# The first batch's down projection of a finished tile, issued two attention units later on TensorE

## The chip, the core and the metric

The kernel runs on one core of a Trainium2 chip. The time is the device time of one execution in microseconds; lower is better. One execution of the kernel before was also recorded by the hardware profiler, and all rows below come from that one.

## The reference

Sliding-window attention with four sink keys, over 2 batches, 8 heads, 768 positions and head size 64, is followed by two token-and-channel mixers. All data is fp32.

```python
keep = is_sink | in_window                       # 4 sinks, window of 128
scores = where(keep, q @ k.T / sqrt(D), -1e9)
a = exp(scores - max); a = a / (sum(a) + 1e-09)
x = a @ v                                        # -> (B, 768, 512)
# first mixer
h = x.T @ U @ V                                  # U: 768 x 32, V: 32 x 768
u = x + h.T
x = u + relu(u @ w_ch1) @ w_ch2
# second mixer
h = relu(x.T @ w_tok1) @ w_tok2
u = x + h.T
out = u + relu(u @ w_ch1) @ w_ch2
```

The "down projection" of this change is the first product of the first mixer, `x.T @ U`, summed over the positions.

## The kernel before

**Tiles and units.** The positions are cut into tiles of 128 rows: six tiles (T = 0 to 5) for the first batch and six for the second. One attention unit is one head of one tile, numbered u = 8 T + h. For the first batch the function `attention(0)` writes, unit by unit, what is issued. In unit u TensorE computes the scores of head u (three products, line 1185), the product of probabilities and values "pv" of head u - 4 (line 1212, four matmul instructions), and the transposes of the probabilities "probsT" of head u - 2 (line 1193). So three heads are in flight. In a unit with h = 0 the queries of the next tile are transposed first, in one with h = 2 its keys (line 1170).

**The other engines in a unit.** VectorE adds the mask and takes the maximum (line 951). ScalarE takes the exponential (line 800). GpSimd copies the sink columns (line 718). The transposed probabilities are copied from PSUM to SBUF, into `probs_T`, by VectorE for even heads (line 962) and by ScalarE for odd ones (line 808). pv of a head waits for that copy.

**The end of a tile.** The last pv of tile T - 1 is issued in unit h = 3 of tile T, and the sink product that completes its output (line 1221) in unit h = 4. VectorE then adds a small number to the eight row sums (line 973), takes reciprocals (line 975) and multiplies the output by them into `x_nat` (line 978). In the same unit VectorE has, ahead of this, the rounding of the next tile's keys (line 935, not in T = 5, where it comes later) and the mask of head 4, and behind it the copy of the transposed probabilities of head 2. At tile T = 3 two more steps on `V_sb` (lines 984 and 987) stand between line 978 and that copy. GpSimd computes the low part of the keys, `k_lo` (line 501), at about the same time.

**The down projection.** In unit h = 5 of tile T, behind everything else of the unit, TensorE multiplies the finished tile T - 1 by U (line 1230, one f32 product that the hardware runs as two weight loads and two matmuls). It waits for `x_nat` of that tile (line 1229). The six products of the first batch add up in one PSUM bank; only the last is followed by anything on another engine (lines 762 and 899). That last one, for tile 5, comes after all attention units of the batch.

**Order of the work.** The list `plan` holds one order for all engines; each engine walks it and issues its own part of each step. The step `("down", 1, 0, t)` with t below 5 makes TensorE issue its product and makes no other engine, and no DMA queue, do anything. PSUM banks, semaphore values and DMA issues are derived from the same list.

**After the attention.** From about 81 us of the span to its end TensorE does the channel products of the mixers, with the second batch's attention put between them.

Of the kernel before, what the change touches and what calls it, by code (L numbers as in the profile page):

```python
# [5 lines left out]
def attention_then_two_mixers(  # L6
# [57 lines left out]
    def attention(b):  # L64

        lo, hi = b * NQ * H, (b + 1) * NQ * H
        units, late = [], []
        LAG_T, LAG_V = LAGS[b]
        for u in range(lo, hi + LAG_V):
            T, h = divmod(u, H)  # L70
            now, scores, probsT, pv = [], [], [], []
            if u == 0:
                now += [("qT", T), ("kT", T), ("qsplit", T), ("ksplit", T)]
            if lo <= u - LAG_V < hi and (u - LAG_V) % H == H - 1:
                now.append(("sinksT", (u - LAG_V) // H))
            if u == hi and T < NTILES:
                now.append(("ksplit", T))
            if u == hi + 1 and T < NTILES:
                now.append(("ksplit_odd", T))
            if u < hi and T + 1 < NTILES:  # L80
                if h == 0:
                    now.append(("qT", T + 1))
                if h == (2, 1)[b]:
                    now += [("kT", T + 1), ("qsplit", T + 1)]
                if h == 4 and T + 1 < hi // H:
                    now.append(("ksplit", T + 1))
                if h == 6 and T + 1 < hi // H:
                    now.append(("ksplit_odd", T + 1))
            if u < hi:
                scores.append(("scores", u))  # L90
            if lo <= u - LAG_T < hi:
                probsT.append(("probsT", u - LAG_T))
            if lo <= u - LAG_V:
                pv.append(("pv", u - LAG_V))
            sinkpv = [("sinkpv", (u - LAG_V) // H)] if lo <= u - LAG_V and (u - LAG_V) % H == H - 1 else []
            if b == 0 and u < hi + LAG_V - 1:
                pv, late = late + pv, sinkpv
            elif b == 0:
                pv = pv + late + sinkpv
            now += scores + pv + probsT  # L100
            if b == 0 and h == 5 and T > 0:
                now.append(("down", 1, b, T - 1))
            units.append(now)
            if b and sinkpv:
                units.append(sinkpv)
        return units
# [73 lines left out]


    plan = [s for unit in attention(0) for s in unit] + [("down", 1, 0, NQ - 1)]
    waiting = attention(1) + preparation(1, 1)
    for n, s in ((24, ("wload", 0)), (23, ("wload", 1)), (19, ("wsum", 0)), (16, ("wsplit", 0)), (11, ("wsum", 1)),
                 (11, ("wload", 2))):
# [1200 lines left out]
```

How the kernel before makes its waits and increments, by code:

```python
        def wait_drained(eng, s):  # L520
            kind, at = s
            if kind == "qT":
                eng.wait_ge(q_copied, at + 1)
            elif kind == "kT":
                eng.wait_ge(k_copied, at + 1)
            elif kind == "sinksT":
                eng.wait_ge(psinkT_ready, at + 1)
            elif by_act(at):
                eng.wait_ge(probsT_by_act, (at + 1) // 2)
            else:
                eng.wait_ge(probsT_by_dve, at + 1 - (at + 1) // 2)
# [1 line left out]
        def wait_used(eng, c):  # L534
            s = chunks[c][0]
            if s[0] == "mm1":
                eng.wait_ge(m_ready, m_at[s, 0] + 1)
            elif s[0] == "up":
                eng.wait_ge(m_ready, m_at[s[:4], KD - 1] + 1)
            elif s[0] == "down" and s[3] == NQ // 2 - 1:
                eng.wait_ge(m_ready, m_at[s[:3], KG - 1] + 1)
            elif s[0] == "mm2" and ends(s):
                eng.wait_ge(m_ready, m_at[s[:4], TPH - 1] + 1)
            else:
                eng.wait_ge(chunk_done, chunk_count[c])
# [33 lines left out]
            def load_qk(T):  # L580
                if T >= 2:
                    sp.wait_ge(tp_ready, tp_at["kT", T - 2] + 1)
                sp.dma_start(q_nat[:, T % 2, :].rearrange("p (h d) -> p h d", h=H), heads(q, T)) \
                  .then_inc(q_loaded[T % 2], 16)
                sp.dma_start(k_nat[:, T % 2, :].rearrange("p (h d) -> p h d", h=H), heads(k, T)) \
                  .then_inc(k_loaded[T % 2], 16)
```

## Time and profile before

| what | value |
|---|---|
| median of 3 runs | 655.9 us (655.68, 655.9, 657.08) |
| the profiled execution, its own time | 657.41 us |
| its span, first to last instruction | 655.6 us |
| TensorE busy with matmuls | 631.2 us, 96% of the span |
| mean granted TensorE clock | 0.997 |
| first batch's attention, up to its last down projection | about 81 us |

The profiled execution is 1.81 us longer than its span; that is what lies around the first and last instruction. It is 1.5 us longer than the median of the three runs. The span shows which engine waited for which, in rows that give a start, a length and, in brackets, the idle time of the engine just ahead of the instruction with what ended it. The granted clock is a share of 2.4 GHz.

### The profile page before, as it was taken

To read this page: it belongs to the slowest core of one execution; us is meant where nothing else is said; L and a number is where in the kernel's file an instruction comes from. 1 tells how busy PE (TensorE), PEld (TensorE's weight loads), DVE (VectorE), ACT (ScalarE), POOL (GpSimd) and SP (SyncE) were. 2 spreads that over 40 slices of the span, in tenths; PEclk is the share of its full clock that TensorE was granted. 3 is DMA by queue.
4 is the path that set the end of the run, shared out by engine and by line. 5 is a ranking of instruction groups with operands and counts; after the bars stand their busy time and mean duration, and the time that the engine had idled before them with its cause. 6 is when DMAs were issued, how large, how long until landed. Compare 5 with 4: busy or idle time off the path is not lost.

```text
span 655.6 us, 10345 instructions
## 1 busy us (share of the span) xinstructions
PE 631.2 (96%) x3532; PEld 565.9 (86%) x3532; DVE 336.7 (51%) x733; ACT 316.2 (48%) x707; POOL 367.0 (56%) x373
## 2 busy tenths in 40 slices
PE   6888999999999999999999999999999999999998
PEld 5878888889888987799999988889998888899986
DVE  7776552433333254276757562186758325676411
ACT  4655575455444553464545444364544445554321
POOL 8544366656464656246656745375656543757262
PEclk9998999999999999999999999999999999999999
DMA  8344244433324425223232243233232343431142
GB/s 182 85 93 113 50 129 118 110 102 108 97 67 107 148 65 146 64 67 110 81 106 88 70 135 101 81 112 97 81 108 87 103 136 98 134 94 47 49 130 95
DMA packets 88276, 65.51 MB, mean 100 GB/s; under 512 B 43008, under 2 KB 72192, under 8 KB 88224
## 3 DMA queue, kind: packets, MB, share of 16 engines
q1 hardware_dynamic: 88224, 64.85, 35.0%
q8 instruction: 29, 0.48, 0.3%
q14 instruction: 23, 0.19, 0.1%
HBM read 61.42 MB, written 3.15 MB: 98 GB/s over the span
## 4 chain that ended last, share of the span: by engine, by line
PE 87%; DVE 5%; ACT 3%; POOL 2%; issue 2%; DMA 0%; DVEq 0%; ACTq 0%; POOLq 0%
PE bank L1356 33%; PE bank L1155 21%; PE bank L1322 10%; PE bank L1212 4%; PE bank L1185 4%; PE bank L1193 3%; PE bank L1286 3%; PE bank L1249 2%; PE bank L1230 2%; PE bank L1170 1%; PE bank L1263 1%; POOL w_lo L753 1%; ACT w_hi L774 1%; PE bank L1348 1%; DVE x_nat L978 1%
## 5 line engine op out<-in xcount | busy, mean ns | idle before, releaser
L753 POOL TENSOR_TENSOR w_lo<-w_raw,w_hi 128x512 fp32r<-128x512 f32 (+1 forms) x158 | 205.9, 1309 | 170.5 <-ACT w_hi L774 170.0
L774 ACT ACTIVATE w_hi<-w_raw 128x512 fp32r<-128x512 f32 (+1 forms) x158 | 96.3, 618 | 61.0 <-PE bank L1356 43.0
L1155 PE MATMUL bank<-b_hi,a_hi 128*128 128x384 f32 x280 | 94.8, 338 | 1.0 <-DVE temps L1065 0.6
L1155 PE MATMUL bank<-b_lo,a_hi 128*128 128x384 f32 x280 | 94.8, 339 | 0.0
L1356 PE MATMUL bank<-w_hi,hid_hi 128*128 128x512 f32 x216 | 87.6, 406 | 0.0
L800 ACT ACTIVATE probs<-masked,neg_max 128x264 f32<-128x264 f32 x96 | 49.5, 516 | 74.3 <-DVE neg_max L951 73.8
L1356 PE MATMUL bank<-w_hi,hid_lo 128*128 128x512 f32 x216 | 85.1, 394 | 0.0
L1356 PE MATMUL bank<-w_lo,hid_hi 128*128 128x512 f32 x216 | 84.7, 392 | 0.0
L1356 PE MATMUL bank<-w_hi,y_hid 128*128 128x512 f32 x216 | 71.1, 394 | 0.2
L951 DVE CUSTOM_DVE_ANT_0 masked<-bank,masks 128x264 f32<-128x264 f32 x96 | 41.2, 430 | 39.4 <-PE bank L1185 35.5
L718 POOL COPY p_sink<-probs 128x12 f32<-128x12 f32 x96 | 19.3, 202 | 69.8 <-ACT probs L800 68.2
L896 DVE SCALAR_TENSOR_TENSOR hid_lo<-bank,hid_hi 128x384 fp32r<-128x384 f32 x32 | 17.8, 557 | 76.9 <-ACT hid_hi L762 76.9
L1155 PEld LDWEIGHTS bank<-b_hi,a_hi 128*128 128x128 f32 x280 | 52.6, 188 | 3.4 <-POOL a_lo_odd L743 1.0
L1155 PEld LDWEIGHTS bank<-b_lo,a_hi 128*128 128x128 f32 x280 | 52.7, 188 | 1.6
L1212 PE MATMUL bank<-v_nat,probs_T 128*128 128x64 f32 x352 | 51.1, 264 | 1.2 <-ACT probs_T L808 0.7
L1212 PEld LDWEIGHTS bank<-v_nat,probs_T 128*128 128x128 f32 x352 | 48.8, 193 | 2.9 <-ACT probs_T L808 1.8
L1356 PEld LDWEIGHTS bank<-w_hi,y_hid 128*128 128x128 f32 x216 | 40.5, 188 | 9.5 <-POOL w_lo L753 1.5
L1356 PEld LDWEIGHTS bank<-w_hi,hid_lo 128*128 128x128 f32 x216 | 40.5, 188 | 9.0
L1155 PE MATMUL bank<-b_hi,a_lo_even 128*128 128x384 f32 x140 | 47.3, 338 | 0.0
L1155 PE MATMUL bank<-b_hi,a_lo_odd 128*128 128x384 f32 x140 | 47.1, 336 | 0.0
L1356 PEld LDWEIGHTS bank<-w_lo,hid_hi 128*128 128x128 f32 x216 | 40.7, 188 | 7.2 <-issue 0.5
L1356 PEld LDWEIGHTS bank<-w_hi,hid_hi 128*128 128x128 f32 x216 | 40.7, 188 | 6.8 <-POOL w_lo L753 0.3
(137 smaller groups left out, 1410.0 us busy)
## 6 DMA issues: line engine op xcount, KB each, us to landing
w_raw<-in_moe_w_ch_dram SPq DMA_DIRECT2D x144, 256.0 KB, 2.7
w_raw<-in_moe_w_ch_dram SPq DMA_DIRECT2D x20, 512.0 KB, 3.5
q_nat<-in_q_dram SPq DMA_DIRECT2D x12, 256.0 KB, 3.0
k_nat<-in_k_dram SPq DMA_DIRECT2D x12, 256.0 KB, 3.7
v_nat<-in_v_dram SPq DMA_DIRECT2D x12, 256.0 KB, 3.4
out_dram<-o_stage SPq DMA_DIRECT2D x12, 256.0 KB, 3.6
w_raw<-in_moe_w_tok_dram SPq DMA_DIRECT2D x6, 256.0 KB, 2.7
w_raw<-in_moe_w_tok_dram SPq DMA_DIRECT2D x8, 192.0 KB, 2.3
```

Source lines behind the costliest of these rows:

```text
L718: nc.gpsimd.tensor_copy(p_sink[:, T % 2, :].rearrange("p (c n) -> p c n", c=3)[:, :, N_SINK * h:N_SINK * (h + 1)], probs[:, u % 4, P:BLK]. ...
L753: nc.gpsimd.tensor_tensor(w_lo[:, split % NW, 0:n], w_raw[:, split % NR, 0:n], w_hi[:, split % NW, 0:n].bitcast(f32), ALU.subtract) \
L774: nc.scalar.activation(w_hi[:, split % NW, 0:n], w_raw[:, split % NR, 0:n], ACT.Copy) \
L800: nc.scalar.activation(probs[:, u % 4, :], masked[:, u % 3, :], ACT.Exp, bias=neg_max[:, u % (2 * H):u % (2 * H) + 1], scale=-1.0, accum_o ...
L951: nc.vector.tensor_tensor_reduce(out=masked[:, u % 3, :], in0=s_slots(u)[0][:, 0:NK], in1=masks[:, mask_of(T), :], scale=1.0, scalar=3.0e3 ...
L1155: last = mm(bank[:, 0:HALF], w[at % 2][:, a, k, :], u[:, b_part, k, :], start=(first and n == 0), stop=(n == 5), skip_group_check=True)
L1185: last = mm(bank[:, 0:NK], qs[:, T % 2, h // 2, :], keys(ks, T, h // 2, h % 2), start=(n == 0), stop=(n == 2))
L1193: last = nc.tensor.transpose(tp_banks[tp_bank_of[s]][:, j * P:(j + 1) * P], probs[:, u % 4, col:col + P], ident[:, :])
L1212: last = mm(o_bank(T)[:, h * D:(h + 1) * D], probs_T[:, u % 2, j * P:(j + 1) * P], v_nat[:, tile % 3, h * D:(h + 1) * D], start=(h == 0 an ...
L1286: last = mm(m_tile((s[:4], d))[:, 0:HALF], tok[:, g, rows], w[:, slot, 0:HALF], start=False, stop=(g == KG - 1 and n == 2), skip_group_che ...
L1322: last = mm(m_tile(use)[:, 0:HALF], w[:, slot, rows], u[:, kk, cols], start=(n == 0), stop=(n == 3 * KD - 1))
L1356: last = mm(m_tile(use)[:, :], stationary, w[:, slot, :], start=False, stop=(final and n == 2), skip_group_check=True)
```

## The change

The step `("down", 1, 0, T - 1)` is appended to unit h = 7 of tile T in place of unit h = 5. It concerns the five products for tiles 0 to 4, issued during tiles 1 to 5. The sixth keeps its place. Nothing else is edited.

```diff
             now += scores + pv + probsT
-            if b == 0 and h == 5 and T > 0:
+            if b == 0 and h == 7 and T > 0:
                 now.append(("down", 1, b, T - 1))
             units.append(now)
```

## Rows read from the trace of the kernel before

**Rows 1.** The page: TensorE's busy time; shares of the chain that ended last.

```profile
PE 631.2 (96%) x3532; PEld 565.9 (86%) x3532; DVE 336.7 (51%) x733; ACT 316.2 (48%) x707; POOL 367.0 (56%) x373
...
PE 87%; DVE 5%; ACT 3%; POOL 2%; issue 2%; DMA 0%; DVEq 0%; ACTq 0%; POOLq 0%
```

**Rows 2.** Waits of TensorE, 0 to 185 us: total us, times, longest.

```profile
PE bank L1230 <- DVE x_nat L978: 5.4, 5, 1.4
```

**Rows 3.** Timeline of tile 2, units 5 to 8: start, length, engine, line, operands.

```profile
34.68 1.27 POOL L501 TENSOR_TENSOR k_lo<-uT_full,k_hi 64x512 fp32r<-64x512 f32 x1
...
34.80 1.18 DVE L973 TENSOR_SCALAR sums_eps<-sums 128x8 f32<-128x8 f32 x1
...
35.26 0.39 PE L1193 MATMUL bank<-ident,probs 128*128 128x128 f32 x2
...
36.25 0.69 DVE L978 TENSOR_TENSOR x_nat<-bank,recip 128x512 f32<-128x512 f32 x1
36.86 0.41 DVE L962 COPY probs_T<-bank 128x256 f32<-128x256 f32 x1
...
36.99 1.10 PE L1230 MATMUL bank<-x_nat,U_sb 128*96 128x512 f32 x2 [1.35 <-DVE x_nat L978]
...
38.17 0.36 ACT L808 ACTIVATE probs_T<-bank 128x256 f32<-128x256 f32 x1
...
38.30 0.55 PE L1212 MATMUL bank<-v_nat,probs_T 128*128 128x64 f32 x4
...
38.69 0.39 PE L1193 MATMUL bank<-ident,probs 128*128 128x128 f32 x2
...
39.28 0.55 PE L1212 MATMUL bank<-v_nat,probs_T 128*128 128x64 f32 x4
...
39.67 0.39 PE L1193 MATMUL bank<-ident,probs 128*128 128x128 f32 x2
...
39.90 0.60 PE L1170 MATMUL bank<-ident,q_nat 128*128 128x128 f32 x4
```

**Rows 4.** Timeline of tile 5, from unit 5, and the units behind it.

```profile
72.65 0.39 PE L1193 MATMUL bank<-ident,probs 128*128 128x128 f32 x2
...
74.10 0.55 PE L1212 MATMUL bank<-v_nat,probs_T 128*128 128x64 f32 x4
...
76.69 0.66 PE L1212 MATMUL bank<-v_nat,probs_T 128*128 128x64 f32 x4 [0.21 <-ACT probs_T L808]
...
77.19 0.39 PE L1193 MATMUL bank<-ident,probs 128*128 128x128 f32 x2
...
78.76 0.19 PEld L1221 LDWEIGHTS bank<-v_sink,p_sinkT 96*128 96x128 f32 x1 [0.19 <-DVE p_sinkT L967]
```

**Rows 5.** Timeline of tile 1, units 5 to 8.

```profile
24.37 0.39 PE L1193 MATMUL bank<-ident,probs 128*128 128x128 f32 x2
...
25.10 0.41 DVE L962 COPY probs_T<-bank 128x256 f32<-128x256 f32 x1
...
26.41 0.36 ACT L808 ACTIVATE probs_T<-bank 128x256 f32<-128x256 f32 x1
...
28.20 0.60 PE L1170 MATMUL bank<-ident,q_nat 128*128 128x128 f32 x4
```

**Rows 6.** Timeline of tile 4, unit 5.

```profile
62.68 1.10 PE L1230 MATMUL bank<-x_nat,U_sb 128*96 128x512 f32 x2 [1.35 <-DVE x_nat L978]
```

**Rows 7.** Timeline of tile 3, units 5 and 6.

```profile
48.68 1.10 PE L1230 MATMUL bank<-x_nat,U_sb 128*96 128x512 f32 x2 [1.32 <-DVE x_nat L978]
...
50.10 0.42 DVE L962 COPY probs_T<-bank 128x256 f32<-128x256 f32 x1
...
50.58 1.07 PE L1212 MATMUL bank<-v_nat,probs_T 128*128 128x64 f32 x4 [0.43 <-DVE probs_T L962]
```

**Rows 8.** Stretches with busy us (count) of each engine, granted clock, DMA share, GB/s.

```profile
50.60:50.70 0.10, 0.10 (x1) 0.10 (x1) 0.10 (x1) 0.00 (x0) 0.00 (x0) 0.78 0.00 0
...
54.00:54.10 0.10, 0.10 (x2) 0.10 (x1) 0.00 (x0) 0.10 (x1) 0.10 (x1) 0.66 0.00 0
```

## The prediction

> **What bounds the kernel now.** I read the page first. TensorE is busy for 96% of the span and makes up 87% of the chain that ended last [rows 1], so the time changes only where TensorE gains or loses idle time. The list of TensorE's waits comes next: the down projection of line 1230 waits for VectorE's `x_nat` for 5.4 us in five places, the largest single entry of the attention stage [rows 2]. One of the five is the last product (tile 5's), which does not move. The other four are in tiles 1 to 4. In tile 5 there is no wait. It looks as if moving the product behind two more units frees some 4.5 us. Whether it does is to be read from the timeline around each place: what does TensorE meet next when it no longer stops there?
>
> **One place in full: tile 2 [rows 3].** VectorE works in order. It finishes `x_nat` at 36.94 (36.25 + 0.69), and directly behind it stands the copy of the transposed probabilities of head 2, from 36.86 to 37.27. TensorE has ended unit 5 with the transposes at 35.26 and waits from there for `x_nat`, until 36.99. But the pv of head 2 is in unit 6, and it needs that copy. So with the product gone from unit 5, TensorE issues the three score products of unit 6 and then stops for the copy, which comes 0.33 us after the `x_nat` that it had waited for. The wait changes its name and place, and the product that stood beside VectorE's work no longer does.
>
> Step by step. The distance from one unit's transposes to the next pv is 0.59 us (38.69 to 39.28). From a pv that did not wait to its unit's transposes it is 0.39 (38.30 to 38.69). From a pv that waited it is 0.50 (76.69 to 77.19 [rows 4]). Where the down projection stands between transposes and pv, the distance is 1.45 (72.65 to 74.10 [rows 4]); it costs 1.45 - 0.59 = 0.86 us of TensorE when nothing waits. TensorE resumes 0.05 us after the end of what it waited for (36.94 to 36.99).
>
> - Before: pv of head 2 at 38.30, pv of head 3 at 39.28, transposes at 39.67, next tile's queries at 39.90 [rows 3].
> - After: the natural time for pv of head 2 is 35.26 + 0.59 = 35.85; the copy allows 37.27 + 0.05 = 37.32. Its transposes are at 37.82. The pv of head 3 could start at 38.41, but it needs ScalarE's copy, which ends at 38.53 (38.17 + 0.36). That copy is not earlier than before: it stands behind the exponential of head 5, and this behind the mask that VectorE does after the copy of head 2. So pv of head 3 is at 38.58, its transposes at 39.08, then the down projection, and the queries at 39.08 + 0.23 + 0.86 = 40.17, where 0.23 is the distance 39.67 to 39.90.
>
> That is 0.27 us later than before. The bounds: if resuming costs nothing over the plain 0.39, it is 0.05; if ScalarE's and VectorE's copies each came another 0.2 late, some 0.5.
>
> **The other four places.**
> - Tile 4 has the same wait of 1.35 us and the same pattern [rows 6]: +0.27.
> - Tile 1 [rows 5]: VectorE's copy ends at 25.51, so pv of head 2 at 25.56, transposes 26.06, pv of head 3 naturally at 26.65, by ScalarE's copy (26.41 + 0.36) at 26.82, transposes 27.32, queries at 28.41. Before they were at 28.20: +0.21.
> - Tile 3 [rows 7]: here even the kernel before waits for the copy, 0.43 us behind the down projection and the scores, and starts pv at 50.58. The product is wholly beside VectorE's work. After the change pv still starts at 50.58, and the 0.86 us come on top: +0.86. At half clock it would be up to 1.7, but see below.
> - Tile 5 [rows 4]: no wait for `x_nat`, so nothing is gained or uncovered in unit 5. The product moves into the thin units behind unit 47, which have no scores and some short waits: 0.21 us for ScalarE's copy at 76.69, and 0.19 for the sink product's weights at 78.76. If both are filled the end is 0.4 earlier. But the last heads' copies and the sink chain move with the scores, and I find only the first part usable: -0.1. On the other side all of 0.86 could come on top.
>
> Nothing else moves: no other engine and no DMA queue issues anything for these steps. The load of queries and keys waits for transposes that shift by 0.3 us at most per tile. From 81 us on TensorE is the bound until the end, so what is lost by then stays.
>
> Sum: 0.21 + 0.27 + 0.86 + 0.27 - 0.1 = +1.5 us. Its ends, place by place, are about +0.8 and +2.7. Against the profiled execution's own time: 657.41 + 1.5 = 658.9.
>
> **The clock, and the median.** TensorE's granted clock falls to one half (1.2 GHz) at 50.66 and is back to 2.4 GHz at 54.07 [rows 8]. Ahead of it TensorE was idle for 1.32 us, worked for about 1.5, and was idle for 0.43 [rows 7]. In this stretch of 3.41 us TensorE has work all the time, so the fall costs about half, 1.7 us (1.7 of 655.6 is also all that the mean clock of 0.997 leaves room for, so it is the only fall). The profiled execution lies 1.5 us above the median 655.9, and one of the three runs (657.08) lies 1.2 above it. I read this as runs with the fall and runs without it. After the change TensorE has, from 48.68 - 1.32 = 47.36 on, only the three score products of unit 6 (some 0.4 us) before 50.58: one idle stretch of 2.8 us, where there were two with work between. I expect the fall in most runs, no longer in some. Then the median goes from a run without to a run with it: 655.9 + 1.5 + 1.2 to 1.5 gives 658.6 to 658.9. A fall that begins during the idle time costs less, since a part of it is spent waiting; I take 658.5. If half or more of the runs are spared, the median is 655.9 + 1.5 = 657.4.
>
> The Trainium skill speaks against the change here: in "TensorE: Matmul & The Clock Gate", section "HAM oscillation — how this bites in real kernels", it says that waits between bursts of matmuls throttle the clock, and that the next burst starts at the low rate. By it the fall comes with the longer idle time, and the sum is the one with 1.7 us in each run; the trace agrees so far, in that its one fall, at 50.66, follows this very place [rows 8].
>
> **Rivals.**
> - *The wait goes and none takes its place* (faster). TensorE would run through unit 6, and of the 5.4 us [rows 2] all but the last product's share would be gained, about 4.6 us, so 657.4 - 4.6 = 652.8, or 651.3 against the median. It is decided by one thing: whether the copy of head 2 ends before the natural time of its pv (35.85 in tile 2). For it: the list of waits names `x_nat` alone, and in tile 5 TensorE meets no wait in this stretch. Against it: the copy ends at 37.27, behind `x_nat` in VectorE's order, 1.4 us too late. A smaller form, a net gain through VectorE and ScalarE running up to 0.9 us further ahead of TensorE afterwards, would need later waits to fill, and in tiles 1 to 4 there are none. Together 7%.
> - *VectorE's chain itself shortens.* Line 973 takes 1.18 us where GpSimd's `k_lo` runs from 34.68 to 35.95; it ends with it [rows 3]. If the two no longer met, everything from `x_nat` on would be 1 us earlier in three tiles: 658.9 - 3 = 655.9. But nothing ahead of unit 5's end changes, so they meet as before. 3%. The Trainium skill, "SBUF — State Buffer", section on the single rule, calls this an exclusive lock of a shared port pair; whichever begins first holds it.
> - *Same losses, fall of the clock no more frequent than before*: 657.4 by the median, about +0.23%. 25%.
> - *The product adds almost nothing*, because the copies resume faster and tile 5's tail takes it: +0.8, 656.7. 10%.
> - Forecast, 658.5: 55%.
>
> **Chances.** A measurement of this kernel can tell about 0.2% (1.3 us) from no change. Faster than that: 0.07. Within: the small rivals, and a part of the third, together 0.18. Slower: 0.75. The range that should hold 8 of 10: from 656.5 (losses near their low end, clock spared) to 659.6 (losses at 2.2 and the fall in all).
>
> **What would show it.** In the changed kernel's trace line 1230 waits for `x_nat` only once, at the end of the batch. Line 1212 waits for line 962's copy: about 0.6 us in tile 1, 1.4 in tiles 2 and 4, 2.8 in tile 3, and shortly for ScalarE's copy one unit later. The last down projection starts about 1.5 us later than in the trace before, at equal clock. TensorE's busy sum does not change but for the clock. I am wrong if pv of head 2 does not wait in unit 6, if the queries of the next tile come earlier than in the rows above relative to the transposes of unit 5, or if tile 3's stretch costs nothing.

## The result

| | median | runs | mean clock of the runs |
|---|---|---|---|
| before | 656.02 us | 655.68 to 657.08 | not listed here, 0.997 in the profiled one |
| changed | 660.66 us | 660.37 to 661.31 | 0.995 in all six |

The ratio is 1.0068, with a 95% interval of 1.0055 to 1.0081: the changed kernel is slower, by 4.6 us. I had said 658.5, slower by 2.5; the sign was right, the size too small, and the time lies outside my range of 656.5 to 659.6. The profiled executions stand at 657.41 and 660.71 us (spans 655.6 and 658.9), 3.3 apart.

The page of the changed kernel has the same two rows as [rows 1]: TensorE busy for 96%, and 87% of the chain.

```profile
PE 633.5 (96%) x3532; PEld 567.2 (86%) x3532; DVE 336.9 (51%) x733; ACT 316.3 (48%) x707; POOL 366.9 (56%) x373
...
PE 87%; DVE 5%; issue 3%; POOL 2%; ACT 2%; DMA 0%; DVEq 0%; ACTq 0%; POOLq 0%
```

TensorE's waits in the changed kernel, 10 to 86 us (total, times, longest), answer to [rows 2]. The name has changed and the total has grown: the kernel before waited 5.4 us for `x_nat` and 0.4 for the copy of line 962, 5.8 together; the changed one waits 7.2 us for the two:

```profile
PE bank L1212 <- DVE probs_T L962: 5.9, 4, 2.9
PE bank L1230 <- DVE x_nat L978: 1.3, 1, 1.3
```

Tile 2 of the changed kernel, against [rows 3]. TensorE waits in unit 6 for the copy behind `x_nat`, then for ScalarE's copy, and the product now costs its full length between 39.33 and 40.41:

```profile
36.50 0.69 DVE L978 TENSOR_TENSOR x_nat<-bank,recip 128x512 f32<-128x512 f32 x1
37.11 0.41 DVE L962 COPY probs_T<-bank 128x256 f32<-128x256 f32 x1
...
37.58 0.66 PE L1212 MATMUL bank<-v_nat,probs_T 128*128 128x64 f32 x4 [1.33 <-DVE probs_T L962]
...
38.42 0.36 ACT L808 ACTIVATE probs_T<-bank 128x256 f32<-128x256 f32 x1
...
38.83 0.52 PEld L1212 LDWEIGHTS bank<-v_nat,probs_T 128*128 128x128 f32 x4 [0.21 <-ACT probs_T L808]
...
39.33 0.39 PE L1193 MATMUL bank<-ident,probs 128*128 128x128 f32 x2
...
39.56 1.02 PE L1230 MATMUL bank<-x_nat,U_sb 128*96 128x512 f32 x2
...
40.41 0.60 PE L1170 MATMUL bank<-ident,q_nat 128*128 128x128 f32 x4
```

Tile 3 of the changed kernel, against [rows 7]: one idle stretch of 2.87 us.

```profile
51.10 0.66 PE L1212 MATMUL bank<-v_nat,probs_T 128*128 128x64 f32 x4 [2.87 <-DVE probs_T L962]
```

The end of the batch, first in the kernel before, then in the changed one. The view shows GpSimd's second k_lo pair as one row. It is a short operation of 0.27 us (at 78.66, now at 79.71) and a long one of 1.26 us (at 79.00, now at 80.06). Before, line 973 is over at 78.96, 0.04 us ahead of the long one. In the changed kernel it begins at 80.59, inside the long one, and lasts until that ends (80.06 + 1.26 = 81.32; 80.59 + 0.76 = 81.35), 0.54 us longer than before:

```profile
78.66 1.61 POOL L501 TENSOR_TENSOR k_lo<-uT_full,k_hi 64x48 fp32r<-64x48 f32 x2 [0.17 <-POOL k_lo L501]
78.74 0.22 DVE L973 TENSOR_SCALAR sums_eps<-sums 128x8 f32<-128x8 f32 x1
...
79.36 0.69 DVE L978 TENSOR_TENSOR x_nat<-bank,recip 128x512 f32<-128x512 f32 x1 [0.17 <-PE bank L1221]
...
80.11 1.10 PE L1230 MATMUL bank<-x_nat,U_sb 128*96 128x512 f32 x2 [0.85 <-DVE x_nat L978]
```

```profile
79.71 1.61 POOL L501 TENSOR_TENSOR k_lo<-uT_full,k_hi 64x48 fp32r<-64x48 f32 x2 [0.17 <-POOL k_lo L501]
...
80.59 0.76 DVE L973 TENSOR_SCALAR sums_eps<-sums 128x8 f32<-128x8 f32 x1
...
81.63 0.69 DVE L978 TENSOR_TENSOR x_nat<-bank,recip 128x512 f32<-128x512 f32 x1
...
82.37 1.53 PE L1230 MATMUL bank<-x_nat,U_sb 128*96 128x512 f32 x2 [1.26 <-DVE x_nat L978]
```

The clock of the changed kernel, against [rows 8]. The column ahead of the last two is the granted clock. It falls to one half at 52.2 and is back at 55.6, and it falls a second time, from 82.9 to 86.3:

```profile
52.10:52.20 0.10, 0.10 (x3) 0.04 (x1) 0.10 (x1) 0.10 (x2) 0.00 (x0) 0.91 0.00 0
55.50:55.60 0.10, 0.10 (x2) 0.08 (x1) 0.00 (x0) 0.00 (x0) 0.00 (x0) 0.53 0.00 0
82.90:83.00 0.10, 0.10 (x2) 0.10 (x1) 0.00 (x0) 0.00 (x0) 0.00 (x0) 0.51 0.00 0
86.30:86.40 0.10, 0.10 (x2) 0.10 (x2) 0.00 (x0) 0.00 (x0) 0.10 (x1) 0.93 0.00 0
```

**Where the 3.3 us are.** The start of the query transposes (line 1170) is a mark in each tile; its distance from one tile to the next compares executions whatever their offset.

| us from mark to mark | before | changed | difference | forecast |
|---|---|---|---|---|
| tile 1 | 11.44 | 11.64 | +0.20 | +0.21 |
| tile 2 | 11.70 | 11.97 | +0.27 | +0.27 |
| tile 3 | 13.80 | 15.11 | +1.31 | +0.86 |
| tile 4 | 11.88 | 11.99 | +0.11 | +0.27 |
| tile 5, to the last down projection | 14.53 | 14.86 | +0.33 | -0.1 |
| from there to the next mark (83.41; 87.00) | 3.30 | 4.63 | +1.33 | 0 |

With 0.04 us of offset at the start the sum is 3.6; of this the later stage gives back 0.3 (why was not looked into). In the kernel before, tile 4 still has 0.19 us of the clock's fall in it: without one, tiles 3 and 4 last 12.79 and 11.69 us (the trace with tile 5 alone moved, below). So tiles 3 and 4 together held 1.20 us of the fall before and 1.5 after, beside the product's 0.86 and tile 4's 0.25.

### The profile page after: what moved, and what is told of

It is laid out like the page before. It is cut to its first block, busy times and chain, and to the rows that moved or that the text cites. A ratio compares the mean times of both kernels' runs of the same rounds, so it can differ in the third digit from the quotient of the medians.

```text
span 658.9 us, 10345 instructions
## 1 busy us (share of the span) xinstructions
PE 633.5 (96%) x3532; PEld 567.2 (86%) x3532; DVE 336.9 (51%) x733; ACT 316.3 (48%) x707; POOL 366.9 (56%) x373
## 4 chain that ended last, share of the span: by engine, by line
PE 87%; DVE 5%; issue 3%; POOL 2%; ACT 2%; DMA 0%; DVEq 0%; ACTq 0%; POOLq 0%
PE bank L1356 33%; PE bank L1155 21%; PE bank L1322 10%; PE bank L1212 4%; PE bank L1185 4%; PE bank L1193 3%; PE bank L1286 3%; PE bank L1249 2%; PE bank L1230 2%; PE bank L1263 2%; PE bank L1170 1%; POOL w_lo L753 1%; PE bank L1348 1%; DVE sums_eps L973 1%; DVE masked L951 1%
```

## The experiments

The clock is listed for each run. It sorts the runs of the kernel before into three groups, over the 69 runs beside the experiments: about 655.9 us at a mean clock of 1.0 (27 runs), 656.2 at 0.999 (16), and 657.2 at 0.997 (25); one is at 0.992. Below, "full clock" means runs at 1.0. One fall of 3.41 us at half clock takes 0.0026 off the mean. Two falls give 0.995. The changed kernel was measured ahead of the experiments and not beside them, so e5, e6, e9 and e13 are compared with runs of another time; the kernel before, measured beside each group, had medians of 656.06 to 656.31 us.

**Parts of the change (e1 to e4).** The condition differs:

```diff
-            if b == 0 and h == 5 and T > 0:
+            if b == 0 and T > 0 and h == (7 if T == 3 else 5):          # e1
+            if b == 0 and T > 0 and h == (7 if T == 5 else 5):          # e2
+            if b == 0 and T > 0 and h == (5 if T == 5 else 7):          # e3
+            if b == 0 and T > 0 and h == (7 if T in (1, 2, 4) else 5):  # e4
```

> The product stands in unit 7 for tile 3 alone, the other four stay in unit 5. My theory: the 0.86 us of the product come on top, since pv of head 2 starts at the same time as before, and the one idle stretch of 2.8 us makes the clock fall in every run: about +0.9 us against an execution of the kernel before that has the fall, +2.3 to 2.6 against one without. No second fall near the end of the batch. Rival (the clock does not matter, the loss is the same 0.6 to 0.9 us in each tile): +0.9 against the median before.

Measured: 659.05 us, ratio 1.0037 (1.0024 to 1.005). No run is at full clock: three have one fall (658.9), two have two. The direction is as forecast, and there is a fall in every run; against runs of before with one fall it is +1.6, not +0.9. The marks say why: tiles 3 and 4 last 14.82 + 12.20 = 27.02 us, 2.54 more than without a fall, which is 0.86 for the product and 1.68 for a fall that begins only after TensorE is at work again (52.5 to 55.95). The fall of the kernel before costs 1.20: a part of it passes in short waits for ScalarE's copy. The rival is refuted.

> The product stands in unit 7 for tile 5 alone. Theory A, the second fall of the clock near 83 us of the changed kernel comes from the thin units behind unit 47 being pushed apart by this product: the fall is here too, and the time is +1.5 to 2 us against before. Theory B, the fall comes from elsewhere: no fall at the end, and between 0 and +0.4 us, of which 0.4 would be line 973 held by GpSimd's k_lo as in the changed kernel.

Measured: 657.62 us, ratio 1.0014 (1.0001 to 1.0027). Four of ten runs are at full clock, at 656.3, so tile 5's move alone costs 0.4 us; the marks give 14.86 against 14.53, with line 973 at 0.76 us. Six runs have one or two falls, and the trace has one, from 80.2 to 83.6. Half of A and half of B: the lock and the fall are two things, and both were seen with this move.

> The product stands in unit 7 for tiles 1 to 4, tile 5 keeps unit 5. Theory A (the second fall comes of tile 5's move): one fall only, and 660.7 less 1.3 for the fall and less 0.2 to 0.4 for the tail: 658.9 to 659.2. Theory B: two falls and 660.2 to 660.7.

Measured: 659.76 us, ratio 1.0058 (1.0039 to 1.0077), in a wide spread: 658.8 to 662.8. The trace (661.0 us of span) is one at a mean clock of 0.99 and shows three falls, the first twice as long as the others. One begins at 67.2, in tile 4, where of all the other traces only that of e13 has one. And one is at the end of the batch although tile 5 isn't moved:

```profile
50.10:50.20 0.10, 0.00 (x0) 0.00 (x0) 0.10 (x1) 0.00 (x0) 0.00 (x0) 0.61 0.00 0
56.90:57.00 0.10, 0.10 (x3) 0.10 (x2) 0.00 (x0) 0.10 (x1) 0.00 (x0) 0.76 0.00 0
67.10:67.20 0.10, 0.10 (x4) 0.10 (x3) 0.06 (x2) 0.04 (x2) 0.10 (x1) 0.94 0.86 266
70.60:70.70 0.10, 0.10 (x2) 0.10 (x2) 0.00 (x0) 0.10 (x1) 0.00 (x0) 0.99 0.00 0
84.20:84.30 0.10, 0.00 (x0) 0.00 (x0) 0.10 (x1) 0.00 (x0) 0.10 (x1) 0.78 0.00 0
87.60:87.70 0.10, 0.10 (x2) 0.10 (x1) 0.10 (x1) 0.10 (x2) 0.00 (x0) 0.66 0.00 0
```

So theory A as I had it, that only tile 5's move brings a fall at the end, is wrong. The median lies between the two forecasts, in neither.

> The product stands in unit 7 for tiles 1, 2 and 4. My theory: +0.20, +0.27, +0.27 = +0.7 us at equal clock, with line 1212 waiting for the copy of line 962 by 0.4, 1.3 and 1.3 us and line 1230 waiting in tile 3 alone. Rival (the loss is all of the clock): 0.

Measured: 658.18 us, ratio 1.0023 (1.001 to 1.0036); at full clock (three of ten runs) 656.8, +0.9 against 655.9. The trace has no fall, and its marks give +0.19, +0.28 and +0.25. Its waits of TensorE, 10 to 75 us:

```profile
PE bank L1212 <- DVE probs_T L962: 3.5, 4, 1.3
PE bank L1230 <- DVE x_nat L978: 1.3, 1, 1.3
```

The mechanism in these tiles is as forecast. But seven of ten runs have falls here too.

**The length of the idle time (e5, e9).** In e5 the rounding of V and its low part leave the end of tile 2's output and stand beside units 25, 27 and 31, the second in two halves:

```diff
-                    if T == 2:
-                        ... # V3_sb high and low parts, lines 983 to 988
+                if s == ("pv", 21):
+                    ... # high part
+                elif s in (("pv", 23), ("pv", 27)):
+                    ... # low part, one half of the columns each
```

> The changed kernel (all five products in unit 7) with the two steps on V_sb taken out of tile 3's end of tile and put, in three pieces, beside units 25, 27 and 31. My theory: tile 3 becomes a place like tiles 2 and 4, line 1212 waits there for 1.3 us instead of 2.9, the clock doesn't fall there: 660.7 - 1.5 - 1.7 = 657.5, and still no faster than before. Rival (the length of the idle stretch is not what brings the fall): fall as before, 659.

Measured: 659.05 us, ratio 1.0041 (1.0024 to 1.0057). The longest wait of line 1212 (here 1214) is 1.8 us instead of 2.9, not the 1.3 that I expected, and the kernel is 1.6 us faster than the changed one, but a fall at 50.0 us stays in the trace, and another at 80.7. Shortening the wait by a third wasn't enough; the rival isn't refuted by this run. In e9 the changed kernel fills its waits with useless repetitions:

```diff
-                    for n, (qs, ks) in enumerate(((q_hi, k_hi), (q_hi, k_lo), (q_lo, k_hi))):
+                    for _ in range({(2, 6): 3, (3, 6): 6, (4, 6): 3}.get((T, h), 1)):
+                        for n, (qs, ks) in enumerate(((q_hi, k_hi), (q_hi, k_lo), (q_lo, k_hi))):
+                            ... # the same product as before, one level deeper
```

> The changed kernel, with the three score products of unit 6 issued again and again into the same bank while TensorE would only wait: 5 more times in tile 3, twice more in tiles 2 and 4 (some 0.35 us each time). The result of the scores is the same. Theory (the idle time ahead of the copy is what brings the clock down in tile 3): no fall near 52 us in the trace, the next tile's queries come 1.3 to 1.5 us earlier against those of tile 3, and the median is 1 to 1.5 us under the changed kernel's 660.7. Rival (the fall has nothing to do with this idle time): one or two falls as before, 660.7.

Measured: 658.27 us, ratio 1.0040 (1.0025 to 1.0055), with 27 more matmuls than the changed kernel and 2.4 us less. Three of four runs are at full clock, where none of the changed kernel's is. The clock of the trace in four stretches:

```profile
12.00:30.00 18.00, 16.27 (x118) 14.61 (x118) 13.10 (x48) 11.92 (x40) 10.96 (x21) 1.00 0.56 131
30.00:50.00 20.00, 19.40 (x161) 17.94 (x160) 14.97 (x48) 11.30 (x37) 8.73 (x18) 1.00 0.35 79
50.00:60.00 10.00, 8.84 (x70) 7.61 (x69) 6.31 (x22) 5.83 (x19) 3.59 (x8) 1.00 0.17 39
60.00:90.00 30.00, 27.48 (x203) 23.60 (x202) 19.41 (x60) 17.86 (x54) 13.65 (x24) 1.00 0.31 78
```

This run splits the result. Its tiles last 11.66, 11.96, 13.65, 11.95 and 14.87 us: against the same tiles without a fall that is +0.22, +0.26, +0.86, +0.26, +0.34. That is 1.9 us in all. At full clock the move costs 658.24 - 655.92 = 2.3 us by the runs; of the 0.4 between the two figures 0.25 lies ahead of tile 1's mark in this trace (17.01 against 16.76), and I have no cause for it. The other 2.4 us of the changed kernel are the clock: with its waits cut to 0.59, 1.03 and 0.56 us in tiles 2 to 4, three of four runs have no fall. The trace has none at the end of the batch either, although nothing was filled there and TensorE waits 1.26 us for `x_nat` as in the changed kernel. So that wait alone doesn't bring the second fall.

**Without the product (e10).** The five products are left out, and the sum starts with the last tile:

```diff
-            if b == 0 and h == 5 and T > 0:
-                now.append(("down", 1, b, T - 1))
```

> The kernel before with the first five products of the first batch left out, so the sum over positions has only the last tile in it. Theory: in tiles 2 to 4 TensorE waits for the copy of line 962 instead, as in the changed kernel, so that leaving out 0.86 us of work saves only 0.86 - 0.27 = 0.6 us in tiles 2 and 4, 0.65 in tile 1, nothing in tile 3, 0.5 in tile 5: 655.85 - 2.3 = 653.5 at full clock, 1.2 to 1.5 more with a fall in tile 3, which should be the usual case, and so 654.5 to 655. Rival (the wait for x_nat was the cost): 655.85 - 4.3 - 4.5 = 647.

Measured: 656.17 us, ratio 1.0003 (0.9994 to 1.0013). Leaving five products out saves nothing in the median. The waits, 10 to 86 us, are those of the changed kernel, in a trace whose lines are two lower:

```profile
PE bank L1210 <- DVE probs_T L960: 6.0, 4, 2.9
```

Tiles 1 and 2 are 0.65 and 0.52 us shorter than before, as expected. From the mark of tile 1 to the last mark of the table above, at 82.58 in this trace, it is 65.82 us against 66.65 before, with two falls against one. At 1.3 us for the second fall, some 2.1 us are saved at equal clock; this is an estimate from these marks, near the 2.3 of the theory, and about half of the 4.3 that five products of 0.86 us take. I was too low by 1.2 to 1.7 us since all ten runs have falls, nine of them two or more. The rival of 647 us is far off.

**VectorE's chain (e6, e11, e7, e8).** Lines 973 and 975 move one unit earlier, ahead of the keys' rounding:

```diff
-                elif s[0] == "sinkpv":
+                elif s[0] == "pv" and s[1] % H == H - 1:
+                    T = s[1] // H
                     ... # wait, line 973, wait, line 975
+                elif s[0] == "sinkpv":
```

> The changed kernel with lines 973 and 975 one unit earlier on VectorE, ahead of the keys' rounding, so that they don't meet GpSimd's k_lo. My theory (VectorE's chain up to the copy of head 2 sets the time, wherever the product stands): line 973 takes 0.17 us in every tile, the copy comes 1.3 us earlier in tiles 2 to 4, and the waits of line 1212 are 0.2, 0.1 to 0.3, 1.5 and 0.1 to 0.3 us. Some 654 us, at most one fall. Rival (the wait of line 1212 comes from something else, such as ScalarE's chain): little change, 659 to 660.

Measured: 656.43 us, ratio 1.0003 (0.9989 to 1.0016): 4.2 us faster than the changed kernel, with falls in all ten runs. Tiles 2 and 4 last 10.83 and 10.82 us instead of 11.97 and 11.99. The seven runs with one fall have a median of 656.35, so a second fall isn't what my 654 lacked. Tile 3's wait is 2.1 us, not 1.5, and line 973, which I expected at 0.17 us in every tile, takes 1.01 us at the end of the batch, where it meets GpSimd's k_lo again. Both come on top of what the fall costs.

> The kernel before (products in unit 5) with lines 973 and 975 alone one unit earlier. Theory: waits of line 1230 near 0.2 us in tiles 1 to 4, and 1.3 us earlier after tile 2 and after tile 4, 1.4 after tile 3, where the copy behind V_sb still holds unit 6 by 0.6: 655.85 - 4 = 651.9 or a little above.

Measured: 652.91 us, ratio 0.9954 (0.9939 to 0.9969), all four runs at full clock; I was 1 us too low. Tiles 2 and 4 last 10.54 and 10.57.

> The kernel before (products in unit 5) with both edits, lines 973 and 975 one unit earlier and V_sb moved. Theory: the waits of line 1230 in tiles 1 to 4 go to 0.2 us or less, no fall of the clock: 655.85 without a fall, less 1.37 in tiles 2 and 4, less 1.9 in tile 3, gives 651.2.

Measured: 652.04 us, ratio 0.9934 (0.9917 to 0.9951). Three of four runs at full clock, the fourth at 0.999; I was 0.8 us too low. In its trace line 973 (here 981) takes 0.17 us ahead of k_lo, and the product follows the transposes with a wait of 0.21 us:

```profile
33.40 0.17 DVE L981 TENSOR_SCALAR sums_eps<-sums 128x8 f32<-128x8 f32 x1
...
34.75 1.27 POOL L501 TENSOR_TENSOR k_lo<-uT_full,k_hi 64x512 fp32r<-64x512 f32 x1
...
34.96 0.69 DVE L989 TENSOR_TENSOR x_nat<-bank,recip 128x512 f32<-128x512 f32 x1
...
35.70 1.10 PE L1234 MATMUL bank<-x_nat,U_sb 128*96 128x512 f32 x2 [0.21 <-DVE x_nat L989]
```

> As the run with both edits, but the products in unit 7. Theory: once VectorE's chain is short, the place matters less: by ScalarE's copy of head 3 still some 0.3 to 0.4 us in tiles 2 to 4 and 0.4 in tile 5, so 652.5 to 653. If the place in unit 7 were bad in itself (a queue, the order of banks), it would be 4 us above the one with unit 5, as after against before.

Measured: 653.42 us, ratio 0.9959 (0.9944 to 0.9973), three of four runs at full clock, 0.4 above my 652.5 to 653. Between unit 5 and unit 7 there are 1.4 us left. Both are nearly free of falls, so this stands beside the 2.3 us at full clock (e9) and not beside the 4.6.

> The kernel before (products in unit 5) with the steps on V_sb alone moved to units 25, 27 and 31. Theory: tile 3 becomes like tiles 2 and 4, 0.6 to 0.9 us earlier, and there is no fall, so that nearly all runs lie at 655.0 to 655.4. Rival (V_sb's own 1.5 us on VectorE cost as much elsewhere): 655.9.

Measured: 656.24 us, ratio 1.0003 (0.9992 to 1.0014). At full clock 655.5, so 0.3 to 0.4 us gained, and falls in five of ten runs and partly in two more. Tile 3 gains 0.58 us, near what I expected (12.21 against 12.79), but the falls stay, so most runs miss 655.0 to 655.4: alone the move is worth nothing that the median shows.

**The end of the batch (e13, e14).** Nine transposes of finished tiles are issued ahead of the last down projection:

```diff
                     use = (s[:3], 0)
+                    if (b, t) == (0, NQ - 1):
+                        for d in range(KD - 1):
+                            up_transposes(("up", 1, 0, 0), d)
```

> The changed kernel, with nine of the twelve transposes that follow the last down projection (line 1263) issued ahead of it, where TensorE waits 1.26 us for x_nat. Theory A (waiting at the end of the batch brings the second fall): the wait shrinks to 0.2 us, that gives 1.0, the second fall goes in most runs, that gives 1.3; tile 3's fall stays: 658.3 to 658.6. Theory B (the second fall doesn't hang on this wait, but on the thin units as a whole or on what came before): two falls as before, 659.6.

Measured: 661.07 us, ratio 1.0063 (1.0047 to 1.0079). Three runs have one fall (659.8), three have the equivalent of three (662.0). The trace is of the second kind: no fall at the end, but one of double length at 50.6 and one at 67.7. The last wait for `x_nat` is 0.29 us, near the 0.2 expected. So the fall at the end was absent where the wait was filled, in one trace; how many falls there are in all was not reduced. The median is above both forecasts, and the theories are not told apart.

> The kernel with the products in unit 5, lines 973 and 975 one unit earlier and V_sb moved (652.04), with the nine transposes issued ahead of the last down projection too. TensorE's largest wait that is left, 0.9 us for x_nat at the end, is filled with work of its own: 651.2 to 651.4, no fall.

Measured: 652.17 us, ratio 0.9935 (0.9923 to 0.9947), no better than e7 and 0.8 above my forecast. The first fence is e7's waits of TensorE from 66 to 80 us, the second those of e14. The same thing as in the change itself happens: the wait is taken over by the next instruction that needs the result.

```profile
PE bank L1234 <- DVE x_nat L989: 0.9, 1, 0.9
```

```profile
PE bank L1293 <- DVE low L899: 1.1, 1, 1.1
```

## Why the prediction was right in kind and wrong in size

- *The wait changes its name and place.* Right, in each of four tiles: copy waits of 0.43, 1.33, 2.87 and 1.30 us where I had 0.6, 1.4, 2.8, 1.4. e10 shows it from the other side: with the product gone, the same waits stand there.
- *+0.21, +0.27, +0.27 in tiles 1, 2, 4.* Right: +0.20, +0.27 and +0.25.
- *Tile 3, +0.86 for the uncovered product.* Right at full clock (e9: 13.65 - 12.79). The clock's part grew beside it: 1.20 us before, 1.5 to 1.7 where the fall begins later. I had taken it as equal. The 1.7 that I worked out for the fall before, because TensorE has work all through it, is too much: at full clock the same work has a wait for ScalarE's copy in it (0.34 us ahead of its weight loads in e2), and a part of the fall passes there.
- *Tile 5, -0.1.* Wrong: +0.33. The term for the short waits was right: counted from the tile's mark, line 973 begins 0.08 us earlier than before (13.08 against 13.16) and the sink product 0.07 (13.11 against 13.18). What I left out is the lock. The scores of units 46 and 47 go earlier, and GpSimd's k_lo with them, by 0.88 us, so that its long operation now runs when line 973 is issued. Of the 0.54 us, 0.13 were a wait for the sink product before, and 0.41 are a loss. I had written this lock down as a rival only in the direction of a gain, "nothing ahead of unit 5's end changes, so they meet as before", and not looked at tile 5, where they had missed each other by 0.04 us.
- *One fall, and in most runs.* This is the step that failed, the clock's term in the sum: I let the clock fall once, in tile 3, and priced the change of the median at +1.2 to +1.5 for it. It measured 2.4. All six runs have two falls' worth, and the second costs 1.33 us in the trace. With it and tile 5's 0.43 the profiled sum goes from 1.5 to 3.3, with 0.3 for the clock in tile 3 and 0.3 given back later. By the runs, e9 at full clock is 2.3 above before and the changed kernel 2.4 above that; together they make the median's 4.6. So the terms beside the clock, 1.5 in my sum, were 0.8 too small, and the clock's 0.9 to 1.2.
- *The reading of the median as runs without a fall, and of 657.08 and 657.41 as runs with one*: right, by the clocks listed with later runs (655.9 at 1.0, 657.2 at 0.997).

Shown: the transfer of the wait; what the uncovered product costs; that the changed kernel with filled waits runs mostly without a fall (three of four runs against none of six; few runs, but e10, measured beside e9 with its waits unfilled, has falls in ten of ten). Not settled: which wait brings the second fall. The wait at the end of the batch is not enough for it: e9 has all of it and no fall in its trace. It came at the end of the batch in the traces of the changed kernel, e2, e3, e5, e8 (at 76.9), e10 and e12, and not in those of before, e1, e4, e6, e7, e9, e11, e13 and e14; tile 5's move is in four of the first seven and in three of the other nine. The same program has runs with none and with two, and I did not find an edit that moves this fall alone.

## What to carry to other kernels

When a wait for one result is removed, look up what stands right behind that result on the engine that makes it and who needs that: here it was ready 0.33 us later, so all of the wait stayed and the work that had filled it was laid bare. Cure the chain, not the place of the waiter: taking one 8-column operation out of a lock's way and 1.5 us of one-time work off VectorE's path gave 3.9 us (e7), where moving the waiting product cost 4.6. And where a change lengthens TensorE's waits, price the clock too, at each such place, not only at the one where the trace at hand shows a fall; runs that list their clock tell how often it comes.

## What the runs showed of the hardware

- Useless matmuls in a wait made the kernel faster: 27 more of them, 2.4 us less (e9 against the changed kernel, medians).
- Line 973, a VectorE operation on 8 columns that takes 0.17 us by itself, lasts as long as the GpSimd operation on SBUF that is running when it is issued: 1.17 to 1.18 us in tiles 2 to 4, 0.76 in tile 5 of the changed kernel, 1.01 in e8. The Trainium skill, "SBUF — State Buffer", section "Who interferes with whom", the single rule, describes this as an exclusive lock of the port pair that the two engines share, and these traces agree. Not every small operation is held: in tile 1 of the changed kernel line 975, the reciprocal of the same 8 columns, took 0.20 us from 24.29 while GpSimd's k_lo ran from 24.17 to 25.44.
- A stretch at half clock lasted 3.41 us in the trace before, and twice that, 50.1 to 57.0, in e3; the first cost 1.2 us, part of it passing in short waits, and the one of e1, which began behind them, 1.7.
